# Whole 64x64 inverses built a tile ahead, and attention outputs kept by dimension and passed through memory

## The reference

```
k_n = k / (norm(k) + 1e-6)                 # attention: a state D x D for each (b, h)
for t in range(S):
    y[t]  = q[t] @ state
    v_old = k_n[t] @ state
    state = state + beta[t] * outer(k_n[t], v[t] - v_old)
x = y as (B*S = 3072) x (H*D = 384)
h = relu(x @ w_in);  x1 = (h * h) @ w_out                        # 384 -> 2048 -> 384
g = x1 @ w_gate;  out = (silu(g) * (x1 @ w_val)) @ w_out2        # 384 -> 1536 -> 384
```

## Time and profile before

| | before |
|---|---|
| median of 3 runs | 1049.33 us (1049.27 to 1049.44) |
| the profiled execution: its own time | 1047.97 us |
| its span on the core | 1046.3 us |
| TensorE busy | 990.5 us |
| VectorE busy | 408.2 us |
| ScalarE busy | 303.0 us |
| GpSimd busy | 208.1 us |

### The profile page before, as it was taken

One profiled execution on the slowest core, in us unless ns is written; L12 is line 12 of the kernel. 1 busy time (PEld: TensorE's weight loads), 2 busy tenths in 40 slices (PEclk: granted clock), 3 DMA queues, 4 the chain that ended last, 5 costly groups with the idle time before them and its releaser, 6 DMA issues.

```text
span 1046.3 us, 24211 instructions
## 1 busy us (share of the span) xinstructions
PE 990.5 (95%) x10752; PEld 823.0 (79%) x10752; DVE 408.2 (39%) x693; ACT 303.0 (29%) x599; POOL 208.1 (20%) x337
## 2 busy tenths in 40 slices
PE   2189999999999999999999999999999999999998
PEld 2178899788778878878888888888888888888887
DVE  3965644434434434543256521322312311322222
ACT  2225333333323333332245411221212211212121
POOL 1186381028307703820000000000000000000000
PEclk9999999999999999999999999999999999999999
DMA  7656423431452052130044010100100100100000
GB/s 232 189 151 197 143 74 86 131 95 53 110 154 63 26 152 80 52 107 23 2 173 145 15 61 1 50 11 1 61 1 1 61 1 1 61 1 0 31 1 31
DMA packets 74392, 73.88 MB, mean 71 GB/s; under 512 B 53168, under 2 KB 53296, under 8 KB 74288
## 3 DMA queue, kind: packets, MB, share of 16 engines
q1 hardware_dynamic: 68624, 64.99, 21.0%
q10 hardware_dynamic: 5664, 7.34, 2.2%
HBM read 56.59 MB, written 15.73 MB: 69 GB/s over the span
## 4 chain that ended last, share of the span: by engine, by line
PE 83%; POOL 8%; DVE 3%; DMA 3%; issue 1%; SPq 1%; ACT 0%; ACTq 0%; POOLq 0%; DVEq 0%
PE bank L895 82%; POOL tinv L399 4%; POOL prod L396 4%; DVE first_tinv L399 1%; DVE first_prod L396 1%; SPq L415 1%; DMA k_sq<-in_ky 1%; DMA inv_scratch<-tinv 1%; POOL tri L390 0%; DMA k_dim<-in_kt 0%; DMA tri_scratch<-gram 0%; DMA first_tri<-tri_scratch 0%; DVE h_lo L856 0%; PE bank L1024 0%; DMA inv<-inv_scratch 0%
## 5 line engine op out<-in xcount | busy, mean ns | idle before, releaser
L895 PE MATMUL bank<-x_hi,w_hi 128*128 128x512 f32 (+1 forms) x768 | 295.3, 384 | 1.2 <-DVE x_lo L831 1.2
L895 PE MATMUL bank<-x_lo,w_hi 128*128 128x512 f32 (+1 forms) x768 | 289.6, 377 | 0.0
L895 PE MATMUL bank<-x_hi,w_lo 128*128 128x512 f32 (+1 forms) x768 | 289.4, 377 | 0.0
L895 PE MATMUL bank<-h_hi,w_hi 128*128 128x512 f32 (+1 forms) x552 | 210.7, 382 | 2.6 <-DVE h_lo L856 2.5
L895 PE MATMUL bank<-h_hi,w_lo 128*128 128x512 f32 (+1 forms) x552 | 204.8, 371 | 0.0
L895 PE MATMUL bank<-h_lo,w_hi 128*128 128x512 f32 (+1 forms) x552 | 204.8, 371 | 0.0
L874 DVE TENSOR_TENSOR stage<-bank,stage 128x512 f32<-128x512 f32 x72 | 49.8, 692 | 318.5 <-ACT stage L741 318.5
L895 PEld LDWEIGHTS bank<-x_hi,w_hi 128*128 128x128 f32 x768 | 145.2, 189 | 29.4 <-DVE x_lo L831 1.6
L895 PEld LDWEIGHTS bank<-x_hi,w_lo 128*128 128x128 f32 x768 | 145.2, 189 | 26.5
L895 PEld LDWEIGHTS bank<-x_lo,w_hi 128*128 128x128 f32 x768 | 145.4, 189 | 24.9
L850 DVE TENSOR_TENSOR stage<-stage,bank 128x512 f32<-128x512 f32 (+1 forms) x112 | 68.4, 611 | 224.3 <-ACT stage L715 224.2
(11 more groups left out here) (84 smaller groups left out, 576.6 us busy)
## 6 DMA issues: line engine op xcount, KB each, us to landing
w_raw<-in_w SPq DMA_DIRECT2D x12, 576.0 KB, 3.8
k_dim<-in_kt SPq DMA_DIRECT2D x12, 512.0 KB, 4.7
q_dim<-in_qt SPq DMA_DIRECT2D x12, 512.0 KB, 3.8
k_prep<-in_kt SPq DMA_DIRECT2D x10, 512.0 KB, 4.2
x1s<-in_w ACTq DMA_DIRECT2D x12, 384.0 KB, 4.7
k_sq<-in_ky SPq DMA_DIRECT2D x12, 384.0 KB, 3.7
v_tok<-in_vy SPq DMA_DIRECT2D x12, 384.0 KB, 4.0
x_scratch<-x1s SPq DMA_DIRECT2D x18, 256.0 KB, 3.1
```

The source lines that it names most:

```text
L895: return pe.matmul(dst, lhsT, rhs, start=start, stop=stop, **kw)
```

## The change

Tile 0 stays nearly as it is (its Z makes only the 32 rows that are used). From tile 1 on:
- **Whole inverses.** After `solve`, GpSimd also writes a copy of the inverses with rows and columns exchanged (`flipped`, over `tri`), which is stored to `flip_dram`. Inverses and their flips come back into the free right half of `grams` (`load_cross`, six transfers a tile), next to the gram blocks. Stage `N1` (64 products with 32 columns of weights and 32 moving) makes gram block by inverse, ScalarE and VectorE copy it out with its sign changed; `N2` (64 such products) makes the block of the inverse below the diagonal, and `take_whole` copies it into `inv`, one buffer of 32 slots now. `load_diagonal` (four transfers) brings the diagonal blocks. `U` then gives final values; Z and DZ are gone.
- **Ahead.** G of tile t + 2 runs in unit t (slots 9 and 14), lane and solve of tile t + 1 begin at slot 1 (slot 3 in unit 2), N1 of tile t + 1 is in slot 32, N2 in slot 0 of the next unit. For tile 2 they are in slots 1 and 4 of unit 2, for tile 1 in slots 26 and 28 of unit 0.
- **Outputs by dimension.** Y of chunks 2 to 11 has state and u as weights (48 columns) and queries and `qk` moving (64 columns), so it gives 48 dimensions by 64 steps. They go to `y_dim`, by two transfers a chunk to `y_dram`, by one a chunk to `x1s`, and from there into `x_hi` and `x_lo`, one kc at a time, in slots 31, 33 and 33. The transposes are gone, and the next unit waits for each kc by itself.
- **Lanes** are numbered by half first, so that ten loads a tile are enough where eight brought the diagonal blocks alone.
- **Order.** Squares and root of chunk 4 go from unit 0 to unit 1; the triangles of chunk 5 are stored before the inverses of tile 1 are loaded. x1 of a unit is stored by units, one unit earlier.

```diff
-                put(24, "sq", 4)
                 put(24, "KS", 2)
-                put(26, "QK", 2)
-                put(27, "lane", 2)
-                put(28, "U", 2)
-                put(30, "Z", 2)
-                put(31, "root", 4)
-                put(32, "DZ", 2)
+                put(26, "N1", 1)
+                put(28, "N2", 1)
+                put(29, "lane", 2)
+                put(30, "QK", 2)
+                put(32, "U", 2)
             elif u == 1:
...
+                put(6, "sq", 4)
                 put(8, "U", 3)
-                put(11, "Z", 3)
-                put(14, "DZ", 3)
-                put(16, "Y", 3)
-                put(18, "DS", 3)
+                put(9, "root", 4)
+                put(10, "G", 6)
+                put(12, "Y", 3)
+                put(15, "DS", 3)
+                put(18, "G", 7)
...
+                    if t == 2:
+                        put(1, "N1", t)
                     if p < NIT:
-                        put(0, "G", p0)
-                        put(10, "G", p1)
-                        put(16, "lane", p)
+                        put(3 if t == 2 else 1, "lane", p)
+                        put(32, "N1", p)
+                    if t + 2 < NIT:
+                        put(9, "G", 2 * t + 4)
+                        put(14, "G", 2 * t + 5)
+                    put(4 if t == 2 else 0, "N2", t)
-                    chain(n0, dict(KS=2, QK=4, U=5, Z=7, DZ=9, Y=11, DS=12))
-                    chain(n1, dict(KS=14, QK=15, U=17, Z=19, DZ=21, Y=23, DS=24))
+                    chain(n0, dict(KS=2, QK=6, U=8, Y=11, DS=12) if t == 2 else dict(KS=3, QK=5, U=7, Y=10, DS=12))
+                    chain(n1, dict(KS=15, QK=16, U=18, Y=21, DS=23))
-                    for g in range(4):
-                        put(30 + g // 3, "X", t, g)
+                    for kc in range(KC):
+                        put(31 + 2 * (kc > 0), "X", t, kc)
...
+                elif name == "N1":
+                    pe.wait_ge(blocks_loaded, 96 * n)
+                    for m in range(16):
+                        for s in range(2):
+                            for bp in range(2):
+                                block = grams[n % 2][late(bp), s, m // 8, m % 8, :]
+                                done = mm(pair[bp][early(bp ^ s), m * HALF:(m + 1) * HALF], block[:, 0:HALF], block[:, HALF:C])
...
+                                        mm(pair[r ^ flip][dims(ab), at:at + C], state[dims(r), m, :], q_dim[dims(r), m, :],
...
+                elif name == "X" and n > 0:
+                    act.wait_ge(x_loaded, 32 * n)
+                    act.wait_ge(up_filled, NF1 * (n + 1))
+                    copy(x_hi[:, kc, :].rearrange("p (s t) -> p s t", s=2), x_raw(kc)).then_inc(x_hi_ready, 1)
...
             for u in range(2, NIT):
+                store_x1(u - 1)
                 load_v(n1)
...
                 if p < NIT:
                     load_q(n2)
+                store_y(n1)
                 if p < NIT:
                     store_inverses(p)
                     load_ktok(n2)
-                    load_inverses(p, 0)
-                    load_inverses(p, 1)
+                    load_inverses(p)
+                load_x(n1)
+                if g < NIT:
+                    load_triangles(g)
...
             for t in range(1, NIT):
...
                 solve(pool, t, tri, tinv, prod, sub_step, SUB * (t - 1))
+                pool.tensor_copy(tri[:, :, :], tinv[:, :, :].rearrange("p c i -> p i c")).then_inc(flipped, 1)
```

More of the change, by code:

```diff
@@ L143, in program @@
         inv_stored = sem("inv_stored")
+        flipped = sem("flipped")
+        flip_stored = sem("flip_stored")
+        blocks_loaded = sem("blocks_loaded")
+        whole_loaded = sem("whole_loaded")
+        cross_filled = sem("cross_filled")
+        cross_ready = [sem(f"cross_ready{x}") for x in range(2)]
+        whole_filled = sem("whole_filled")
+        whole_ready = [sem(f"whole_ready{ab}") for ab in range(2)]
         first_stored = [sem(f"first_stored{i}") for i in range(3)]
@@ L305, in program @@
         for one in [one for u in range(NIT + 1) for slot in range(SLOTS) for one in PLAN[u].get(slot, [])]:
-            if one[0] in MATMULS:
+            if one[0] in MATMULS and (one[0] != "X" or one[1] == 0):
                 count = 1 if one[0] == "X" else 2
@@ L665, in run @@
                     store_triangles(act, n, 1)
+                elif name == "N1":
+                    act.wait_ge(cross_filled, n)
+                    for bp in range(2):
+                        act.activation(cross_rows(n, 0, bp), blocks(BANKS[stage_][bp][early(0), :]), ACT.Copy, scale=-1.0
+                                       ).then_inc(cross_ready[0], 1)
+                elif name == "N2":
+                    act.wait_ge(whole_filled, n)
+                    take_whole(copy, stage_, 0)
                 elif name == "fetch":
@@ L805, in run @@
                                           mask[:, :].unsqueeze(1).to_broadcast([P, 8, C]), ALU.mult).then_inc(qk_ready, 1)
+                elif name == "N2":
+                    dve.wait_ge(whole_filled, n)
+                    take_whole(copy, stage_, 1)
+                elif name == "N1":
+                    dve.wait_ge(cross_filled, n)
+                    for bp in range(2):
+                        dve.tensor_scalar(cross_rows(n, 1, bp), blocks(BANKS[stage_][bp][early(1), :]), -1.0, None, ALU.mult
+                                          ).then_inc(cross_ready[1], 1)
                 elif name == "KS":
@@ L984, in q_state @@
                                     m = 8 * bp + 2 * a + ab
+                                    if n > 1:
+                                        at = (4 * bp + a) * C
+                                        mm(pair[r ^ flip][dims(ab), at:at + C], state[dims(r), m, :], q_dim[dims(r), m, :],
+                                           start=(flip == 0 and a == 0), stop=False, skip_group_check=True)
+                                        continue
                                     at = (4 * bp + a) * D
@@ L1132 @@
     w_out, w_out2 = inputs["moe_w_out"], inputs["moe2_w_out"]
+    lanes = beta.reshape(2, 2, 4, 2, n // 2, 2, 2, 32)
+    first = lanes.transpose(5, 6, 0, 3, 2, 1, 4, 7).reshape(128, n // 2, 32)
+    later = lanes.transpose(6, 0, 5, 3, 2, 1, 4, 7).reshape(128, n // 2, 32)
     arrays = {
```

276 lines of the change are left out of this document (207 added, 69 removed).

## The result

The changed kernel takes 1035.65 us (median of 4 runs, 1034.42 to 1036.51) against 1049.38 for the kernel before: the ratio is 0.9854, 95% interval 0.9835 to 0.9873, so it is faster by 1.3 to 1.7%. Forecast were 1029.5 us and 19.8 us of gain in a range of 1023 to 1041; 13.7 us came, by the medians. The profiled execution took 1036.29 us with a span of 1034.5, 11.7 less than that of before.

What follows compares the result with a forecast made beforehand. TensorE was taken to bound the kernel over most of the span. Terms of 22.3 us off and 2.5 on gave 19.8 us gained, so 1049.33 - 19.8 = 1029.5 us, with a range of 1023 to 1041.

Steps and rivals of the forecast that it cites:

- units of 86.5 us: Sign expected in the changed profile: units 3 and 4 take 86.5 us where there were 90.
- Transposes: Tiles 1 to 5 lose the transposes (X) on TensorE: 1.6 us a tile, 8.0 us gained in five.
- N1 and N2: Chunks 2 to 11: ten stages N1 and N2 at 1.70 us replace twenty at 1.31; gain 9.2 us.
- The line through 48 and 64 columns: Pace of N1 and N2 extended from two measured weight widths: 1.55 us a stage, gain 10.7 us.
- the proportional rule: N1 and N2 with weight-load time proportional to columns, from the Trainium skill: 1.39 us a stage, gain 12.3 us.
- my step toward a floor: For N1 and N2, 1.70 us a stage was taken, between the line's 1.55 and 1.97 at DS's pace.
- Y, gain 3.5: Y of ten chunks: weights of 48 instead of 64 columns save 0.35 us each, 3.5 us, bounds 0 and 4.2.
- N1's place: N1 in slot 32 delays `h_lo` of block 15; TensorE waits 0.5 us in each of units 2 to 4, 1.5 us.
- Tile 2 late: N1 in unit 2's slot 1: 1.0 us lost, bounds 0 and 6; rival 4 to 8 us more, 1033 to 1037, chance 0.15.
- Slower through `load_x`: Rival: output loads queue behind inverses on SyncE and stop ScalarE in slot 31; 1053 us at 8 each, chance 0.10.
- Small products have a floor: Rival: N stages run at DS's or KS's pace and Y gets no faster; 1033 to 1040 us, chance 0.20.
- small terms: Narrower Z of chunks 0 and 1, 0.6 us; U's wait in unit 5, 0.8; chunk 4's square leaving unit 0, 0.2.

Runs made afterwards that it cites:

- e4_tokens: Changed kernel with outputs by token again (Y, X and copies of the kernel before, no output stores and loads), whole inverses kept; 1043.59 us, ratio 0.9939.
- e2_wide: Changed kernel with 64 instead of 32 columns of weights in N1 and N2, moving side and instruction count unchanged; 1039.82 us in one run.
- e3_y48: Changed kernel whose Y of chunks 2 to 11 moves 48 of the 64 columns, weights still 48 wide; 1034.58 us in one run.
- e9_n1late: Changed kernel with N1 of tiles 3 to 5 in slot 34 instead of 32; 1035.56 us, ratio 0.9852.
- e5_held: Changed kernel with tile 2's triangles loaded first, tile 1's diagonal-block loads and all transfers behind them held until N2 of tile 1 is done; 1032.08 us, ratio 0.9820.
- e6_split: Kernel of e5_held with N1 of tile 1 and every N2 in halves, nine matmuls between, lanes of tiles 4 and 5 one slot later; 1035.53 us, ratio 0.9856.
- e7_order: Kernel of e5_held with QK of chunk 2 between N1 and N2 of tile 1, and U of chunk 2 in slot 33; 1034.88 us, ratio 0.9851.
- e1_hold: Changed kernel with 1.66 MB of SyncE loads (chunks 2, 3, 4 and 6) held until N2 of tile 1 is done; 1035.37 us, ratio 0.9860.
- f_after: Changed kernel with four more 512 KB transfers, DRAM to DRAM, issued by SyncE at the start of unit 5; 1044.51 us in one run.

## Why the prediction was right, and where its steps failed

**Bound and direction: right; the size was 6.1 us too good.** The time followed TensorE's work, and no engine took its place. But 1035.65 us lies outside the 1025 to 1032 that the forecast gave for itself. It lies inside the range only because that had been widened for the floor and for a late tile 2, and neither made the difference: the stops in unit 0 did, which no term and no rival held. That part of being right is luck. Of the signs that it named, units of 86.5 us came in unit 3 (87.0) and not in unit 4 (84.2), because the prediction counted G as only moved and overlooked that unit 4 loses its own.

**Transposes, 8.0: right, a bit large.** `e4_tokens` gives 1.45 to 1.65 a tile for transposes and Y together, 1.3 to 1.5 without Y's 0.16: 6.5 to 7.5 in five.

**N1 and N2, gain 9.2: the size was low.** The run of 1.22 us with 0.23 of switches is 1.45 a stage, ten 14.5, and the gain 11.7. The line through 48 and 64 columns had 1.55, the proportional rule 1.39; the value lies between them, and my step toward a floor was not borne out. `e2_wide` shows that the weights' width is the reason why N is cheaper than Z and DZ were.

**Y, gain 3.5: the step failed.** The sentence "The width of the weights sets the pace of these 64 instructions and the moving width hardly does" holds only while weights have 64 columns. At 48, the moving side of 64 is the limit: 0.8 us came for ten chunks. `e3_y48` shows it.

**N1's place, +1.5: right in mechanism, a bit large.** In the changed kernel (TensorE and VectorE at the end of unit 2):

```profile
267.82 0.39 PE L1059 MATMUL bank<-h_hi,w_hi 128*128 128x512 f32 x1
...
268.06 0.69 DVE L1018 TENSOR_TENSOR h_lo<-stage,h_hi 128x512 fp32r<-128x512 f32 x1 [0.32 <-ACT h_hi L782]
...
268.81 0.50 PE L1059 MATMUL bank<-h_hi,w_hi 128*128 128x512 f32 x1
```

Matmuls three apart stand 0.99 apart instead of 0.69: before the last of them TensorE waits for `h_lo`, which ends at 268.75. That is 0.3 more than normal, 0.9 in three units, of which `e9_n1late` got 0.4 back. Unit 4 has another of 0.5 before the first `h_hi`, not foreseen.

**Tile 2 late, +1.0 and a rival of 0.15: did not happen.** N1 of tile 2 starts at 184.63, right behind the first up group of unit 2 (182.47 + 2.04). In `e5_held`, whose unit 2 begins 1.7 us earlier, there is no wait either.

**Slower through `load_x`, 0.10: did not happen.** ScalarE has no wait for `x1s` loads.

**Small products have a floor, 0.20: not for N**, whose products start 9.5 ns apart; Y's part of that rival came true, for another reason, its moving side. The rival's times were also a little off: 2.7 to 10.4 us less gain is 1032.2 to 1039.9, with the middle at 1036, and the best case of 24.6 adds up (to 24.5) only with both waits at nothing.

**What was missing.** The prediction set the time of SyncE and of the transfers only against the data that stages wait for, and not against the instructions that TensorE itself fetches through the same engines. No term of the sum and no rival held this, and that is the step that failed. That cost 0.5 + 4.5 us of stops in unit 0, about 2.3 us of half clock behind them (4.7 us at half pace), and some 0.85 and 0.17 us in units 2 and 3 (against `e5_held`, where the stop at 6849 is absent and that at 9665 is 0.37 instead of 0.73). With them the sum is: 7.0 (transposes) + 11.7 + 0.8 + 1.6 (small terms as forecast, not measured by themselves) = 21.1 off; 0.9 + 0.5 (`h_lo`) + 4.9 (stops, less normal spacing) + 2.3 + 1.0 + 0.66 (later start of unit 0) = 10.3 on; 10.8 of the 11.7 that the two profiled executions differ by. The other 0.9 is what unit 0 of the changed kernel saved at its start, where the clock was already up (see Open). That the sum closes so well is in part chance: the transposes, the small terms and the clock's share are estimates.

**Open.** Whether block c in unit 0 could be had in time by another order alone was not settled: `e6_split` and `e7_order` moved the wait to U. Why unit 0 in some runs starts at the lower clock (to 70.4 us in the kernel before, 70.7 in `e1_hold`) and in others not was not tried. What it costs can be read: from the first up matmul of unit 0 to instruction 1831, where each trace waits for `h_lo`, the five that start low take 14.8 to 14.9 us and the nine others 13.7 to 14.0. So it is worth about 1 us; the profiled execution of the kernel before paid it and that of the changed kernel did not. How often the unprofiled runs paid it is not known.

## What to carry to other kernels

When a change makes small matmuls cheaper, count instructions per microsecond as well as microseconds: two stages of 256 instructions each within 5.4 us (112.5 to 117.9) outran TensorE's fetch, whose blocks come through the same engines as the data. Keep bursts of transfers away from such stages, by a wait on the stage itself; in `e5_held` that gained 3.6 us. And price a narrow matmul by the longer of its two sides, to within some 15%: the one that had not mattered becomes the limit as soon as the other is cut.

## What the runs showed of the hardware

- TensorE's instructions arrive in transfers of 16384 bytes, 256 instructions; in twelve of the fourteen kernels traced there is a stop of 0.7 us or more at a number 193 over a multiple of 256. With the engines quiet, block c of `e1_hold` began 1.1 us behind the end of the previous stop, took 1.0, and the engine went on 1.4 us behind its end: 3.5 us for a block that N2 uses in 1.2.
- Stops of 4.3 to 5.5 us in all brought 6.8 us of granted clock at 1.2 GHz, those of 2.2 to 3.5 us brought 3.4. But 3.2 us in `e2_wide` brought 6.8, and 4.2 in unit 0 of `f_after` 10.2; where the stop was 1.4 us and the waits after it 0.8 and 2.4 (`e6_split`) there was none. So the length of the stop does not settle it.
- Four tiles of the array in turn: 9.5 ns a weight load and matmul at 32 columns of weights and 32 moving, 15.6 at 64 and 32, 12.2 (Y of `e3_y48`) and 13.6 (DS) at 48 and 48, 15.0 at 48 and 64, 16.9 at 64 and 48, 17.2 at 64 and 64.
